# A threshold mask moved from a Pool compare to an Activation Sign and a Relu, with w_out split on Activation and Pool, and the first tiles and loads reordered

## The chip, the cores and the metric

One core of a Trainium2 chip. The metric is the device time in microseconds (us). TensorE is called PE here, VectorE DVE, ScalarE ACT, GpSimd Pool, and SP is the engine that only starts transfers.

## The reference, cut to what matters

Three layers follow each other: attention in which each row keeps its 32 largest scores, a dense layer pair with a parametric Relu, and a layer of eight experts of which each token takes two.

```
scores = scale * np.matmul(q, k.transpose(0, 1, 3, 2))          # (2, 8, 576, 576)
kth = np.partition(scores, -32, axis=-1)[..., -32:-31]
scores = np.where(scores >= kth, scores, -1e9)
attn = exp(scores - max); attn /= attn.sum(-1) + 1e-9
x = (attn @ v), heads beside each other                         # (1152, 512)
h = x @ w_in                                                    # w_in (512, 2048)
g = np.maximum(h, 0.0) + alpha * np.minimum(h, 0.0)
x = g @ w_out                                                   # w_out (2048, 512)
logits = x @ w_gate; noise_scale = log1p(exp(x @ w_noise))      # 8 experts
out = for each token: its two best experts, weight * (relu(x @ w1[e]) @ w2[e])
```

All is float32.

## The kernel before

**Stages.** The 1152 tokens are nine blocks of 128. In the first stage (to about 466 us) the program walks through 72 tiles: tile 8 * blk + h is head h of block blk, 128 rows by 576 scores. Behind it the routing is worked out and rows are scattered to their experts; the last stage (from about 530 us) runs the experts. The change touches the first stage only.

**One tile.** PE multiplies queries and keys into PSUM (`score_tile`, five tiles ahead of the rest), each number as a high and a low part. ACT copies the scores out (`copy_scores`). DVE works on pairs of tiles (`topk_pair`): four times MAX8 and three times MATCH_REPLACE8 for each tile, interleaved, and one small operation for the negated maxima (`neg_max`). ACT takes exp (`exp_tile`). Pool makes the mask `scores >= top[31]` (L1432) and multiplies it into the exponentials (L1434), both in `probabilities`. PE transposes the product in five pieces (`prob_transpose`, L846 and L848), ACT copies the pieces (`copy_prob_t`), and PE multiplies them with v (`prob_values`, L862). `row_sums` on DVE and `normalise` on Pool divide.

**The dense layers between.** While block blk is in attention, block blk - 1 goes through w_in (`first_layer`, at h = 1 to 4), back transposes (`h_transpose`), the parametric Relu and w_out (`second_layer`, at h = 5, 6, 7 and at h = 0 of the next block), in four chunks of 512. For each chunk ACT takes Relu of the negated and of the plain value (`relu_both`), scales the negated one by minus alpha with four operations of 128 columns (L1193), Pool adds the two (`prelu`, L1447), ACT rounds the sum to its high part (`high_g`), and Pool subtracts (`low_g`, L1452). `prelu` stands at h = 4, 5, 6, 7 of Pool's order.

**Order.** Every engine has its own order, written out by hand as a loop over h = 0 to 7 for each block; blocks 0 to 4 and 8 are written out, 5 to 7 are a loop. Semaphores are the only tie. An engine that waits holds back all that is queued behind it. The scores have eight buffers, exponentials, maxima and thresholds four.

**w_out's parts.** In block 1 DVE splits w_out into high and low, a quarter behind each of the four pairs (`split_w_out`, L389 and L391). w_in is loaded once PE has four tiles of scores, w_out once it has eight.

## Time and profile before

| | us |
|---|---|
| median of 3 runs | 786.79 (786.48 to 788.63) |
| the profiled execution | 789.1 |
| its span | 787.3 |
| mean granted PE clock | 0.952 of full speed |
| busy: PE, DVE, ACT, Pool | 688.5, 567.0, 435.2, 421.4 |

The profile is one execution. A slice of a line of tenths is 19.7 us. "Idle before" is what an engine stood still before an instruction, and behind the arrow stands what released it. The start of a tile's last transpose (L848) marks its place on PE: tile 8 at 70.18, tile 16 at 127.29, tile 24 at 178.33, tile 32 at 228.89, tile 40 at 284.00, tile 48 at 331.16, tile 56 at 378.39, tile 64 at 425.56, tile 71 at 465.66. Blocks thus take 57.1, 51.0, 50.6, 55.1, and then 47.2 us each.

### The profile page before, as it was taken

How to read it: one execution, taken by the hardware profiler on the slowest of the kernel's cores; microseconds unless marked ns; L12 is line 12 of the kernel's file. 1: busy time of each engine (PE TensorE's matmuls, PEld its weight loads, DVE VectorE, ACT ScalarE, POOL GpSimd, SP SyncE). 2: the span in 40 equal slices, each digit the busy share in tenths (PEclk: the TensorE clock that was granted, in tenths of full speed). 3: DMA queues.
4: the chain of work that ended last, by engine and by line, in shares of the span. 5: the costliest groups of instructions: out<-in, count | busy, mean ns of one | idle time of the engine just before them, and what ended most of it. 6: DMA issues, size and time to landing. Idle time of an engine off the chain costs nothing. (4 is left out here: it accounts for less than half of the span.)

```text
span 787.3 us, 13289 instructions
## 1 busy us (share of the span) xinstructions
PE 688.5 (87%) x4516; PEld 534.7 (68%) x4516; DVE 567.0 (72%) x1168; ACT 435.2 (55%) x863; POOL 421.4 (54%) x309
## 2 busy tenths in 40 slices
PE   2565788989999999999999989729999999999993
PEld 2454466667675676766667566518989999999893
DVE  5999999989897889897998904653555545555520
ACT  6643464756885758667666645722535535535511
POOL 3875788697776796978879770630202102112022
PEclk9968899999998999999999999958999999999998
DMA  7595001403402504040160205355267376375322
GB/s 230 211 363 226 15 14 55 148 14 120 129 26 65 165 15 149 14 161 13 60 234 13 95 17 198 135 205 183 69 212 219 115 226 193 121 246 161 121 34 33
DMA packets 36718, 98.87 MB, mean 126 GB/s; under 512 B 10480, under 2 KB 11504, under 8 KB 35184
## 3 DMA queue, kind: packets, MB, share of 16 engines
q1 hardware_dynamic: 32288, 88.31, 32.2%
q0 software_dynamic: 4384, 9.98, 5.7%
q8 instruction: 25, 0.41, 0.2%
q14 instruction: 21, 0.17, 0.1%
HBM read 80.15 MB, written 37.34 MB: 149 GB/s over the span
## 5 line engine op out<-in xcount | busy, mean ns | idle before, releaser
L1432 POOL TENSOR_SCALAR scores<-scores,top 128x576 f32<-128x576 f32 x72 | 129.0, 1792 | 78.1 <-issue 31.9
L1530 POOL DMA_INDIRECT out_dram<-ye,xe x24 | 42.8, 1783 | 216.8 <-ACT ye L1354 211.9
L364 DVE MAX8 top<-rest 128x8 f32<-128x576 f32 x216 | 151.9, 742 | 0.0
L884 PE MATMUL bank<-w_in_sb,x_t 128*128 128x512 f32 x272 | 125.9, 606 | 0.3
L1434 POOL TENSOR_TENSOR expo<-scores,expo 128x576 f32<-128x576 f32 x72 | 107.7, 1496 | 6.0
L370 DVE MATCH_REPLACE8 rest<-top,rest 128x576 f32<-128x576 f32 x144 | 105.4, 737 | 0.0
L912 PE MATMUL bank<-w_out_high,g_parts 128*128 128x512 f32 x288 | 99.3, 406 | 1.2 <-DVE g_parts L566 0.8
L1058 PE MATMUL bank<-w_hi,he_t 128*128 128x512 f32 x256 | 91.9, 400 | 0.0
L573 DVE TENSOR_TENSOR w_lo<-raw,w_hi 128x1024 fp32r<-128x1024 f32 x64 | 77.9, 1225 | 19.5 <-ACT w_hi L1301 18.6
L884 PEld LDWEIGHTS bank<-w_in_sb,x_t 128*128 128x128 f32 x272 | 50.3, 195 | 52.0 <-issue 51.1
L846 PE MATMUL bank<-ident,expo 128*128 128x128 f32 x288 | 49.9, 299 | 36.8 <-POOL expo L1434 30.6
L862 PEld LDWEIGHTS bank<-v,prob_t 128*64 128x64 f32 (+1 forms) x1440 | 56.3, 142 | 37.8 <-issue 25.2
L364 DVE MAX8 top<-scores 128x8 f32<-128x576 f32 x72 | 50.9, 748 | 31.8 <-POOL expo L1434 18.6
L1131 ACT COPY prob_t<-bank 128x512 f32<-128x512 f32 x72 | 42.4, 589 | 56.4 <-PE bank L848 56.3
L862 PE MATMUL bank<-v,prob_t 128*64 128x65 f32 (+1 forms) x1440 | 71.7, 238 | 1.5 <-ACT prob_t L1132 1.4
L809 PE MATMUL ps_scores<-k_parts,q_high 128*128 128x288 f32 x160 | 57.4, 372 | 17.2 <-DVE q_low L441 6.3
L1044 PE MATMUL ps_scores<-xe_t,w_hi 128*128 128x320 f32 x320 | 71.4, 310 | 0.0
L1301 ACT CAST w_hi<-raw 128x1024 fp32r<-128x1024 f32 x64 | 66.3, 1045 | 0.2
L846 PEld LDWEIGHTS bank<-ident,expo 128*128 128x128 f32 x288 | 33.3, 150 | 46.7 <-POOL expo L1434 25.3
L912 PEld LDWEIGHTS bank<-w_out_high,g_parts 128*128 128x128 f32 x288 | 55.5, 193 | 13.8 <-POOL g_parts L1452 1.8
L625 DVE SCALAR_TENSOR_TENSOR he_t<-ps_scores,he_t 128x64 fp32r<-128x64 f32 x80 | 22.2, 320 | 52.8 <-ACT he_t L1347 52.8
L1347 ACT ACTIVATE he_t<-ps_scores 128x320 fp32r<-128x320 f32 x40 | 17.5, 439 | 76.2 <-PE ps_scores L1044 76.2
(178 smaller groups left out, 1505.9 us busy)
## 6 DMA issues: line engine op xcount, KB each, us to landing
raw<-w_dram SPq DMA_DIRECT2D x64, 512.0 KB, 9.5
x_sorted_dram<-x_sorted_dram SPq DMA_DIRECT2D x7, 2570.0 KB, 10.8
q_raw<-q_rows_dram SPq DMA_DIRECT2D x18, 256.0 KB, 2.6
xe<-x_sorted_dram SPq DMA_DIRECT2D x8, 514.0 KB, 4.3
w_in_sb<-w_in_dram SPq DMA_DIRECT2D x4, 1024.0 KB, 8.3
w_out_raw<-w_out_dram SPq DMA_DIRECT2D x4, 1024.0 KB, 8.6
out_dram<-x_now SPq DMA_DIRECT2D x1, 3584.0 KB, 30.1
x_sorted_dram<-x_now SPq DMA_DIRECT2D x1, 2570.0 KB, 20.5
```

Of the source, the lines that this page charges most:

```text
L364: nc.vector.max(dst, src).then_inc(chain if r < ROUNDS - 1 else dve_top, 1)
L370: nc.vector.match_replace(rest[:, k, :], top[:, (n + k) % 4, 8 * r:8 * r + 8], src, LOWEST).then_inc(chain, 1)
L573: nc.vector.tensor_tensor(w_lo[par][:, at], raw[par][:, at], w_hi[par][:, at].bitcast(F32), ALU.subtract).then_inc(dve_wl, 1)
L846: pe.transpose(ps_pt[:, kt * P:(kt + 1) * P], expo[:, h % 4, kt * P:(kt + 1) * P], ident[:, :])
L862: mm = pe.matmul(ps_o[lo:hi, c:c + VCOLS], prob_t[0:n, h % 2, kt * P + lo:kt * P + hi], v[0:n, head, kt, :], start=(kt == 0), stop=(kt == ...
L884: mm = pe.matmul(dst, x_t[:, k, :], w_in_sb[:, k, c * 512:(c + 1) * 512], start=(k == 0), stop=(k == MK - 1))
L912: mm = pe.matmul(ps_y[:, :], g_parts[:, c % 2, a, k * P:(k + 1) * P], w[:, at], start=(c == 0 and k == 0 and a == 0 and w is w_out_high), ...
L1044: mm = pe.matmul(h_bank[m % 3][:, 0:GROUP], w[:, k, at], xe_t[:, a, k, :], start=(k == 0 and a == 0 and w is w1_hi), stop=(k == MK - 1 and ...
L1058: mm = pe.matmul(y_bank[t][:, :], he_t[:, m, at:at + P], w[:, m, :], start=(m == 0 and a == 0 and w is w2_hi), stop=(m == EK - 1 and a == 1))
L1301: nc.scalar.copy(w_hi[par][:, at], raw[par][:, at]).then_inc(act_wh, 1)
L1432: nc.gpsimd.tensor_scalar(mask, mask, top[:, n % 4, TOPK - 1:TOPK], None, ALU.is_ge).then_inc(pool_mask, 1)
L1434: nc.gpsimd.tensor_tensor(expo[:, n % 4, :], mask, expo[:, n % 4, :], ALU.mult).then_inc(pool_prob, 1)
```

## The change

- **Mask.** Pool works out, once for each pair of tiles, minus the next number below the 32nd largest score (`thresholds`: two small tensor_scalar and two small tensor_tensor, three waits between them). ACT writes Sign(score - that number) over the scores (`sign_tile`), for tiles h + 1 and h + 2 at odd h, right behind `copy_prob_t`. Pool keeps one multiplication for a tile; the product is negative where the mask is out. `copy_prob_t` uses Relu in place of Copy, so these become 0.
- **exp.** ACT issues exponentials in pairs at even h, for tiles h + 2 and h + 3.
- **Parametric Relu.** The four scalings by minus alpha move from ACT to Pool, ahead of the addition in `prelu`.
- **w_out.** The high parts are ACT casts at tiles 2 to 9, the low parts Pool subtractions at tiles 5 to 12, in eighths. DVE has none.
- **DVE.** `neg_max` and the row sums' addition become tensor_tensor with a constant operand. A pair starts with its first tile's scores, and waits no longer for Pool's product, but for ACT's exp and for the thresholds of the pair two before it.
- **Start.** Queries are loaded first and cast on DVE; ACT's order in the first tiles changes, and the first exponentials come earlier.
- **Loads.** w_out is loaded at once behind v, w_in when PE has eight tiles of scores, and alpha, gates and noise behind w_in.

```
-                wait(dve, pool_prob, tile - 2)
+                dve.wait_ge(act_scores, tile + 1)
+                wait(dve, act_exp, tile - 2)
+                wait(dve, pool_thr, pairs - 1)
...
-                        nc.vector.tensor_scalar(neg_max[:, m:m + 2], top[:, m:m + 2, 0], -1.0, None,
-                                                ALU.mult).then_inc(dve_negmax, 1)
+                        nc.vector.tensor_tensor(neg_max[:, m:m + 2], zeros[:, :], top[:, m:m + 2, 0],
+                                                ALU.subtract).then_inc(dve_negmax, 1)
...
-                    if split:
-                        split_w_out(pair)
...
+            def high_w_out(c):
+                act.wait_ge(w_out_in[c // 2], 16)
+                at = slice(c * 2 * MODEL, (c + 1) * 2 * MODEL)
+                nc.scalar.copy(w_out_high[:, at], w_out_raw[:, at]).then_inc(act_w_high, 1)
+
+            def sign_tile(tile, n, pairs):
+                act.wait_ge(pool_thr, pairs)
+                act.wait_ge(act_exp, tile + 1)
+                nc.scalar.activation(scores[:, n % SBUFS, :], scores[:, n % SBUFS, :], ACT.Sign,
+                                     bias=neg_below[:, n % 4:n % 4 + 1]).then_inc(act_sign, 1)
...
-                for k in range(4):
-                    ins = nc.scalar.activation(neg[:, c % 2, k, :], neg[:, c % 2, k, :], ACT.Copy,
-                                               scale=neg_alpha[:, 4 * c + k:4 * c + k + 1])
-                ins.then_inc(act_scaled, 1)
...
+                    if h % 2 and not (last and h + 2 >= HEADS):
+                        sign_tile(tile + 1, h + 1, PAIRS * blk + (h + 1) // 2 + 1)
+                        sign_tile(tile + 2, h + 2, PAIRS * blk + (h + 1) // 2 + 1)
...
+            def thresholds(n, pairs):
+
+                pool.wait_ge(dve_top, 2 * pairs)
+                plain(pool)
+                m = n % 4
+                thr = top[:, m:m + 2, TOPK - 1]
+                nc.gpsimd.tensor_scalar(step_up[:, :], thr, NEXT, 0.0, ALU.mult, ALU.max).then_inc(pool_step, 1)
+                nc.gpsimd.tensor_scalar(step_down[:, :], thr, -NEXT, TINY, ALU.mult, ALU.max).then_inc(pool_step, 1)
+                pool.wait_ge(pool_step, 3 * pairs - 1)
+                nc.gpsimd.tensor_tensor(step_up[:, :], step_up[:, :], step_down[:, :], ALU.add).then_inc(pool_step, 1)
+                pool.wait_ge(pool_step, 3 * pairs)
+                wait(pool, act_sign, 2 * pairs - 4)
+                nc.gpsimd.tensor_tensor(neg_below[:, m:m + 2], step_up[:, :], thr, ALU.subtract).then_inc(pool_thr, 1)
+                pool.wait_ge(pool_thr, pairs)
...
-                mask = scores[:, n % SBUFS, :]
-                nc.gpsimd.tensor_scalar(mask, mask, top[:, n % 4, TOPK - 1:TOPK], None, ALU.is_ge).then_inc(pool_mask, 1)
-                pool.wait_ge(pool_mask, tile + 1)
-                nc.gpsimd.tensor_tensor(expo[:, n % 4, :], mask, expo[:, n % 4, :], ALU.mult).then_inc(pool_prob, 1)
+                pool.wait_ge(act_sign, tile + 1)
+                nc.gpsimd.tensor_tensor(expo[:, n % 4, :], scores[:, n % SBUFS, :], expo[:, n % 4, :],
+                                        ALU.mult).then_inc(pool_prob, 1)
...
-                pool.wait_ge(act_scaled, 4 * j + c + 1)
+                pool.wait_ge(act_relu, 4 * j + c + 1)
+                plain(pool)
+                for k in range(4):
+                    ins = nc.gpsimd.tensor_scalar(neg[:, c % 2, k, :], neg[:, c % 2, k, :],
+                                                  neg_alpha[:, 4 * c + k:4 * c + k + 1], None, ALU.mult)
+                ins.then_inc(pool_scaled, 1)
+                pool.wait_ge(pool_scaled, 4 * j + c + 1)
                 nc.gpsimd.tensor_tensor(pos[:, c % 2], pos[:, c % 2], neg[:, c % 2], ALU.add).then_inc(pool_g, 1)
...
+                    if isinstance(blk, int) and HEADS * blk + h in W_LOW_AT:
+                        low_w_out(W_LOW_AT[HEADS * blk + h])
+                    if h % 2 and not (last and h == HEADS - 1):
+                        thresholds(h + 1, PAIRS * blk + (h + 1) // 2 + 1)
```

DVE between two pairs of block 1, before. `top` holds the largest scores of a row, `rest` the scores with those struck out.

```order
L364 MAX top<-rest 128x8 [waits chain] x2
L389 CAST w_out_high<-w_out_raw 128x2048 [waits w_out_in]
L391 TENSOR_TENSOR w_out_low<-w_out_raw,w_out_high 128x2048 [waits dve_w_high]
L364 MAX top<-scores 128x8 [waits pool_prob,act_scores]
L364 MAX top<-scores 128x8
L370 MATCH_REPLACE rest<-top,scores 128x576 [waits chain] x2
L374 TENSOR_SCALAR neg_max<-top 128x2
```

And the same place after:

```order
L378 MAX top<-rest 128x8 [waits chain] x2
L378 MAX top<-scores 128x8 [waits pool_thr,act_scores,act_exp]
L378 MAX top<-scores 128x8 [waits act_scores]
L384 MATCH_REPLACE rest<-top,scores 128x576 [waits chain] x2
L388 TENSOR_TENSOR neg_max<-zeros,top 128x2
```

The split is gone, and the pair waits for `pool_thr` and `act_exp` in place of `pool_prob`.

Pool at h = 5 and the start of h = 6 of block 1, before; the same order stands in every later block. `expo` are the exponentials, `pos` and `neg` the two halves of the parametric Relu, `g_parts` its high and low part.

```order
L1432 TENSOR_SCALAR scores<-scores,top 128x576 [waits dve_top,act_exp]
L1434 TENSOR_TENSOR expo<-scores,expo 128x576 [waits pool_mask]
L1452 TENSOR_TENSOR g_parts<-pos,g_parts 128x512 [waits act_g_high]
L1447 TENSOR_TENSOR pos<-pos,neg 128x512 [waits act_scaled]
L1432 TENSOR_SCALAR scores<-scores,top 128x576 [waits dve_top,act_exp]
```

And after:

```order
L1469 TENSOR_TENSOR expo<-scores,expo 128x576 [waits act_sign]
L1500 TENSOR_TENSOR g_parts<-pos,g_parts 128x512 [waits act_g_high]
L1491 TENSOR_SCALAR neg<-neg,neg_alpha 128x128 [waits act_relu]
L1491 TENSOR_SCALAR neg<-neg,neg_alpha 128x128 x3
L1495 TENSOR_TENSOR pos<-pos,neg 128x512 [waits pool_scaled]
L1443 TENSOR_SCALAR step_up<-top 128x2 [waits dve_top]
L1444 TENSOR_SCALAR step_down<-top 128x2
L1446 TENSOR_TENSOR step_up<-step_up,step_down 128x2 [waits pool_step]
L1449 TENSOR_TENSOR neg_below<-step_up,top 128x2 [waits act_sign,pool_step]
L1469 TENSOR_TENSOR expo<-scores,expo 128x576 [waits act_sign,pool_thr]
```

One large operation has gone, and four scalings and four threshold operations have come; the next multiplication waits for `act_sign`.

ACT at h = 5 of a block in the loop, before (`h_sb` and `prob_t` are copies out of PSUM):

```order
L1156 COPY h_sb<-bank 128x512 [waits pe_ht1,pe_first]
L1131 COPY prob_t<-bank 128x512 [waits pe_pv,pe_pt]
L1132 COPY prob_t<-bank 64x128
L1200 CAST g_parts<-pos 128x512 [waits pe_second,pool_g]
```

And after:

```order
L1180 COPY h_sb<-bank 128x512 [waits pe_ht1,pe_first]
L1154 ACTIVATE prob_t<-bank 128x512 [waits pe_pv,pe_pt]
L1155 ACTIVATE prob_t<-bank 64x128
L1135 ACTIVATE scores<-scores,neg_below 128x576 [waits act_exp,pool_thr] x2
L1217 CAST g_parts<-pos 128x512 [waits pe_second,pool_g]
```

Two Signs, which wait for the thresholds, stand between the copies and the cast that Pool's `low_g` waits for.

## Rows read from the trace of the kernel before

**Rows 1.** The page, busy tenths of PE and its granted clock in 40 slices:
```profile
PE   2565788989999999999999989729999999999993
...
PEclk9968899999998999999999999958999999999998
```

**Rows 2.** Stretches between last transposes: length, PE, PEld, DVE, ACT, POOL busy, clock, DMA:
```profile
70.18:99.80 29.62, 24.40 (x154) 15.50 (x153) 29.55 (x52) 14.84 (x34) 19.41 (x11) 0.84 0.04 14
99.80:127.29 27.49, 23.23 (x170) 17.25 (x168) 27.38 (x50) 16.00 (x36) 24.41 (x17) 0.94 0.03 11
...
331.16:354.16 23.00, 22.92 (x166) 15.00 (x165) 22.81 (x48) 15.09 (x35) 17.97 (x14) 1.00 0.38 138
354.16:378.39 24.23, 23.05 (x182) 17.25 (x181) 20.02 (x42) 16.85 (x39) 20.76 (x16) 1.00 0.03 11
```

**Rows 3.** Timeline of DVE, block 1: start, us, operation, idle before:
```profile
53.92 1.42 DVE L364 MAX8 top<-scores 128x8 f32<-128x576 f32 x2
...
64.15 1.47 DVE L389 CAST w_out_high<-w_out_raw 128x2048 fp32r<-128x2048 f32 x1
65.65 2.29 DVE L391 TENSOR_TENSOR w_out_low<-w_out_raw,w_out_high 128x2048 fp32r<-128x2048 f32 x1
...
112.94 1.42 DVE L364 MAX8 top<-scores 128x8 f32<-128x576 f32 x2
```

**Rows 4.** Timeline of DVE, the pairs of the first block that waited:
```profile
11.44 1.42 DVE L364 MAX8 top<-scores 128x8 f32<-128x576 f32 x2 [2.85 <-ACT scores L1095]
...
32.80 1.42 DVE L364 MAX8 top<-scores 128x8 f32<-128x576 f32 x2 [1.84 <-ACT scores L1095]
```

**Rows 5.** Groups of Pool from 331.16 to 378.39: busy us, mean ns, idle before:
```profile
L1432 POOL TENSOR_SCALAR scores<-scores,top 128x576 f32<-128x576 f32 x8 | 13.8, 1726 | 7.0 <-issue 4.2 <-ACT expo L1125 2.9
L1434 POOL TENSOR_TENSOR expo<-scores,expo 128x576 f32<-128x576 f32 x8 | 11.3, 1417 | 0.7
L1452 POOL TENSOR_TENSOR g_parts<-pos,g_parts 128x512 fp32r<-128x512 f32 x5 | 6.4, 1281 | 0.5 <-ACT g_parts L1200 0.5
L1447 POOL TENSOR_TENSOR pos<-pos,neg 128x512 f32<-128x512 f32 x4 | 5.2, 1289 | 0.0
```

**Rows 6.** Small Pool operations of the whole span, and ACT's exp, same columns:
```profile
L1387 POOL TENSOR_SCALAR_AFFINE_SELECT ident<-ident 128x128 f32<-128x128 f32 x1 | 0.3, 284 | 0.2 <-POOL ident L1385 0.2
L1475 POOL TENSOR_TENSOR neg_alpha<-below,alpha_sb 128x16 f32<-128x16 f32 x1 | 0.2, 210 | 0.0
...
L1125 ACT ACTIVATE expo<-scores,neg_max 128x576 f32<-128x576 f32 x72 | 55.5, 772 | 0.0
```

**Rows 7.** Timelines of Pool and DVE where small operations of one met the other:
```profile
86.05 1.72 POOL L1432 TENSOR_SCALAR scores<-scores,top 128x576 f32<-128x576 f32 x1
86.27 0.54 DVE L374 TENSOR_SCALAR neg_max<-top 128x2 f32<-128x2 f32 x1
...
338.09 1.41 POOL L1434 TENSOR_TENSOR expo<-scores,expo 128x576 f32<-128x576 f32 x1
338.55 0.97 DVE L374 TENSOR_SCALAR neg_max<-top 128x2 f32<-128x2 f32 x1
...
504.00 0.61 POOL L1511 COPY x<-weight 128x7 f32<-128x7 f32 x1 [2.82 <-DMA x_sorted_dram<-x,slot_i]
503.33 2.36 DVE L573 TENSOR_TENSOR w_lo<-raw,w_hi 128x1024 fp32r<-128x1024 f32 x2
```

**Rows 8.** Timeline of PE and ACT at tile 55 (h = 7):
```profile
371.90 0.66 PE L846 MATMUL bank<-ident,expo 128*128 128x128 f32 x4 [0.89 <-POOL expo L1434]
372.39 0.27 PE L848 MATMUL bank<-ident,expo 128*64 128x128 f32 x1
372.70 0.59 ACT L1131 COPY prob_t<-bank 128x512 f32<-128x512 f32 x1 [1.07 <-PE bank L848]
373.19 0.26 ACT L1132 COPY prob_t<-bank 64x128 f32<-64x128 f32 x1
```

**Rows 9.** Timeline of SP, the issue of w_out's four pieces:
```profile
38.46 2.52 SPq L704 DMA_DIRECT2D w_out_raw<-w_out_dram  x4
```

More of the change, by code:

```diff
@@ L86 @@
 K_LOW_AFTER = {12: (0, 1), 15: (2, 3), 16: (4, 5), 17: (6, 7)}
+W_HIGH_AT = {2 + c: c for c in range(8)}
+W_LOW_AT = {5 + c: c for c in range(8)}
 OTHER_AT = {MIXED * HEADS - AHEAD + i: i for i in range(HEADS)}
@@ L208, in moe_program @@
         dve_k_high = sem("dve_k_high")
-        act_q = [sem(f"act_q{i}") for i in range(2)]
+        q_high_ready = [sem(f"q_high_ready{i}") for i in range(2)]
         q_ready = [sem(f"q_ready{i}") for i in range(2)]
@@ L216, in moe_program @@
         w_in_in = sem("w_in_in")
-        w_out_in = sem("w_out_in")
+        w_out_in = [sem(f"w_out_in{i}") for i in range(4)]
         small_in = sem("small_in")
@@ L346, in _, with topk_pair @@
         def _(dve):
-            def topk_pair(tile, n, mixed=False):
+            def topk_pair(tile, n, pairs, mixed=False):
                 pair = n // 2
-                for k in range(2):
-                    dve.wait_ge(act_scores, tile + k + 1)
-                    if mixed:
-                        dve.wait_ge(act_other, n + k + 1)
-                wait(dve, pool_prob, tile - 2)
+                dve.wait_ge(act_scores, tile + 1)
+                wait(dve, act_exp, tile - 2)
+                wait(dve, pool_thr, pairs - 1)
                 plain(dve)
@@ L361, in topk_pair @@
                             dve.wait_ge(chain, LINKS * pair + 4 * r - 1 + k)
+                        elif k:
+                            dve.wait_ge(act_scores, tile + 2)
+                        if r == 0 and mixed:
+                            dve.wait_ge(act_other, n + k + 1)
+                        if r == 0 and k:
+                            plain(dve)
                         src = rest[:, k, :] if r else scores[:, n + k, :]
@@ L414, in one_block @@
                         row_sums(blk - 1, 0)
-                    if split:
-                        split_w_out(pair)
-                    if pair == (0 if split else 1) and not first:
+                    if pair == (0 if second else 1) and not first:
                         row_sums(blk - 1, 1)
@@ L443, in _ @@
             first_low_keys(1)
+            dve.wait_ge(small_const, 2)
             one_block(0, True)
-            one_block(1, split=True)
+            one_block(1, second=True)
             one_block(2)
@@ L1130, in copy_prob_t @@
                 wait(act, pe_pv, tile - 1)
-                nc.scalar.copy(prob_t[:, n % 2, 0:(KT - 1) * P], ps_pt[:, :])
-                nc.scalar.copy(prob_t[0:LASTK, n % 2, (KT - 1) * P:], ps_pt4[0:LASTK, 0:P]).then_inc(act_pt, 1)
+                nc.scalar.activation(prob_t[:, n % 2, 0:(KT - 1) * P], ps_pt[:, :], ACT.Relu)
+                nc.scalar.activation(prob_t[0:LASTK, n % 2, (KT - 1) * P:], ps_pt4[0:LASTK, 0:P],
+                                     ACT.Relu).then_inc(act_pt, 1)
             def copy_o(blk, n):
@@ L1243, in one_block @@
                         relu_both(blk - 1, TURN_AT[h])
-                    if not (last and h + 2 >= HEADS):
+                    if h % 2 == 0 and not (last and h + 2 >= HEADS):
                         exp_tile(tile + 2, h + 2, PAIRS * blk + (h + 2) // 2 + 1)
+                        exp_tile(tile + 3, h + 3, PAIRS * blk + (h + 2) // 2 + 1)
+                    if isinstance(tile, int) and tile in W_HIGH_AT:
+                        high_w_out(W_HIGH_AT[tile])
                     if isinstance(tile, int) and tile in OTHER_AT:
@@ L1259, in _ @@
             high_keys(0)
-            high_queries(0, 0)
             high_keys(1)
@@ L1273, in _ @@
             high_keys(7)
-            for tile in range(2):
-                exp_tile(tile, tile, 1)
+            sign_tile(0, 0, 1)
+            sign_tile(1, 1, 1)
             one_block(0, mlp=False, gate=False)
@@ L1419, in _ @@
                     pool.wait_ge(q_ready[1], 1)
+                if h == 5:
+                    thresholds(0, 1)
             pool.wait_ge(v_in_first, 32)
```

86 lines of the change are left out of this document (48 added, 38 removed).

## The prediction

> **What bounds the kernel now.** I read the page's tenths first: PE fills all slices but a dip near 500 us from the fifth or sixth on, and the early ones are thin [rows 1]. So the question is which engine holds PE up in which stretch, and the stretches between transposes answer it [rows 2]. In block 1 (70.18 to 127.29, 57.1 us) DVE is busy 29.55 of 29.62 and 27.38 of 27.49 us, while PE does its work at a granted clock of 0.84 and 0.94: DVE bounds. In a block of the loop (331.16 to 378.39, 47.2 us) PE is busy 22.92 of 23.00 and 23.05 of 24.23: PE bounds, and all that a better order can give back is 1.3 us a block. 0.89 of it is one wait, at h = 7, for Pool's product [rows 8]. The second half of that block, h = 4 to 7, is also Pool's fullest: 20.76 of 24.23 us against 17.97 of 23.00 in the first [rows 2]. The change eases DVE and loads just this half.
>
> **The start: -2 us.** The first pair now begins with one tile's scores. Its wait of 2.85 us was for two [rows 4]; the second tile still comes when it came, so one MAX8 of 0.7 us is gained. Pair 2 waited 1.84 us for scores [rows 4], which hung on the first products. Those no longer need the 1.73 us compare, and the exponentials are there earlier. I take all of it: the fifth pair starts at 53.92 [rows 3] less 1.95, 52.0. Bounds are 0 and -2.5.
>
> **Block 1 on DVE.** The four splits cost 1.47 + 2.29 each [rows 3], 15.0 us together, all on the bound, and they go. From 53.92 to 112.94 DVE then needs 59.0 - 15.0 = 44.0 us, 10.6 to 11 a pair: pairs end at 62.7, 73.6, 84.4 and 95.8. If DVE alone counted, tile 16 would be 17 us early.
>
> **neg_max: nothing.** It took 0.97 us when it met Pool's multiply, and ended with it; beside the compare it took 0.54 and ended 0.76 us after the compare began [rows 7]. One could hope that tensor_tensor is free of that. But a Pool copy of 7 elements took 0.61 us while a DVE tensor_tensor ran [rows 7], so I leave the waits in. The Trainium skill says the same of such operations (SBUF: State Buffer, section Who interferes with whom): one with two SBUF inputs contends with a GpSimd instruction that reads SBUF. By that rule the new form waits as the old one did. Were it free, block 1's DVE would end about 1.5 us earlier, and Pool (below) would hide it.
>
> **What Pool gets.** These prices decide.
> - Compare out: 1.73 us a tile, 13.8 us a block [rows 5].
> - Scaling in: 16 tensor_scalar of 128 columns a block. The trace has none. By columns from the compare (1.73 for 576, taken as 0.1 fixed and 2.8 ns a column) one is 0.46 us. Bounds: 0.28, what a one-input 128x128 took [rows 6]; and 1.13, if what the compare did after it let DVE through at 0.76 us (0.97 us more [rows 5, 7]) is a fixed tail: 0.97 + 128/576 of 0.76. I take 0.46, since a tail that long beside 0.28 is odd. One `prelu` goes from 1.29 [rows 5] to 3.13 us.
> - Thresholds in: four operations of two columns, as 0.21 for 16 columns [rows 6], 0.85 us a pair. Bounds 0.4 and, with the fixed tail, 2.4.
> - w_out's low parts in: 1024 columns, twice the 1.28 of 512 [rows 5], 2.55 us, eight times, tiles 5 to 12. The high parts go to ACT, which is busy 14.84 of 29.62 us there [rows 2]: nothing.
>
> **A new wait.** Pool's multiply for an even tile needs ACT's Sign (0.77 as exp [rows 6]), and that needs Pool's thresholds, queued behind `prelu`. With hand-overs, Pool stands still about 0.95 us, before the multiplies of h = 6 and of the next h = 0. On ACT, copy_scores, Relu and the cast for `low_g` are queued behind the waiting Sign; DVE has its scores five tiles ahead, so it does not feel this.
>
> **Block 1 on Pool.** Pair 6 (tile 12) is done at 84.4, thresholds 85.2, Sign 86.2, multiply 87.6. Then Pool has, until tile 16's multiply is done: four `prelu` 12.5, four multiplies 5.7 [rows 5], three `low_g` 3.8, one query part 1.3, the last w_out part 2.55, two thresholds 1.7, two gaps 1.9. Sum 29.5: 117.1. The transposes (0.49 to the start of the last [rows 8]) put tile 16's mark at 117.6 instead of 127.29: **-9.7**. PE's own need from tile 12 on is 23 us [rows 2], so Pool bounds, not DVE.
>
> **Each later block.** PE from tile 3's mark to the next block's tile 0 (h = 4 to 7 and one more step) takes 30.2 us today. After: ACT begins its copies 0.31 behind the mark and needs 0.8 for them [rows 8], then signs tile 4, so Pool's multiply starts 2.0 us behind the mark. From its start to the end of the next tile 0's multiply there are five multiplies 7.1, four `prelu` 12.5, three `low_g` 3.8, query part 1.3, thresholds 1.7, and idle 0.3 + 0.95 + 0.95: 28.6. With the transposes, 31.1, and the block takes 47.2 + 0.9 = 48.1. PE's wait of 0.89 at h = 7 goes to h = 0 and is about twice as long. So:
> - block 2 (tile 16 to 24): 51.0 to 48.1, **-2.9**;
> - blocks 3 and 4 (105.7 us with scores of the second batch, which stretch PE's steps and hide Pool): DVE was late there; **-2**, between -5 and +2;
> - four blocks of 47.2, with the last one shorter: 3.3 x 0.9, **+3**.
>
> **The rest.** w_in is now issued when w_out was, at 38.46 [rows 9]; it is wanted at tile 8, past 62, and w_out's early issue is 30 us ahead of use: nothing, unless a load takes over 20 us. Table and copies with Relu in place of Copy: nothing. The routing and the experts move with tile 71: 0. At the end one `prelu` more of 1.8 us meets a multiply that is 1.1 earlier: 0 to +1.
>
> **Sum.** -9.7 - 2.9 - 2 + 3 = -11.6. Against the profiled execution's 789.1 that is 777.5; against the median of 786.79, which is 0.3% below it, **775.2**.
>
> **Rivals.**
> - *Scaling is costly on Pool* (slower). The price of one 128-column tensor_scalar decides: each 0.1 us more is 1.6 us in the chain of a block, for eight blocks 13 us. From 0.55 us on nothing is gained, and at 0.75 the time is 775 + 38 = 813; with the fixed tail of 1.13 Pool would be busy far beyond 47 us a block, and the time past 860. For it: the compare released DVE at 0.76 and still ran to 1.73 [rows 7]. Against: 0.28 for a one-input 128x128 [rows 6].
> - *Scaling is cheap on Pool* (faster). The compare may be slow as a comparison; a multiplication would then be near 0.28. `prelu` is 2.4 us, a block 46.9, tile 16 comes at 115, limited by PE. -12 - 4 - 3 - 1 = -20: 767. The Trainium skill points here (GPSIMD Engine Reference, section 4.1): one-input operations are roughly line-rate, two-input ones about half as fast. The trace disagrees for the compare, 1.73 against 1.42 of the two-input multiply [rows 5]. Taken fully, it would be this rival's lower end, 762.
> - *The early gain is lost on the way*: tile 16 only 4 us earlier, as ACT's waiting Sign holds up copies or PE's clock stays at 0.84 [rows 2]. 775.2 + 5.7 = 781.
> - That the change does not do what it says is excluded for the splits: their rows are gone from DVE's order.
>
> **Chances.** Forecast (scaling at 0.38 to 0.54) 0.42; cheap 0.18; early gain lost 0.06; costly 0.34. About 0.3% is what a measurement here can tell from no change; of the forecast 0.04 lies within that, and of each of the last two 0.02. Of the lost gain another 0.02 ends slower. So faster 0.38 + 0.18 + 0.02 = 0.58, within 0.08, slower 0.32 + 0.02 = 0.34. The range leaves out some 5% below and 15% above, where the scaling costs over 0.69 us: 763 to 805.
>
> **What would show it.** Right: tile 16's mark at 117 to 118, L1491 at 0.46 us, Pool 24 to 25 us busy in h = 4 to 7, PE's wait at h = 0 on Pool's product, blocks of the loop near 48.1, DVE's neg_max as long as before, the span of the experts unchanged. Wrong: L1491 above 0.55 (the block passes 50) or near 0.3 (PE busy without a gap), or neg_max at 0.15 throughout, or a Sign that waits on DVE.

## The result, and the profile after

The changed kernel takes 830.06 us (median of 4 runs, 826.67 to 830.31) against 787.29 us of the kernel before in the same session: a ratio of 1.0531, 95% interval 1.0500 to 1.0563. It is slower by 5.3%, where 775.2 us and "faster" had been forecast. The profiled execution took 826.67 us, its span is 824.9 us against 787.3.

The page of the changed kernel, the same two lines as in [rows 1], and the shares of its chain that ended last:

```profile
PE   2455987989879989889899898945999999999994
...
PEclk9965899989989999999999999975999999999998
...
PE 48%; POOL 25%; issue 10%; DVE 7%; ACT 6%; DMA 2%; POOLq 0%; SPq 0%; ACTq 0%; DVEq 0%
```

Pool now stands in a quarter of the chain, though it is busy for only 414.0 of 824.9 us. The starts of the last transposes tell where the 37.6 us between the two spans arose. The forecast's steps stand beside them (us, change against the kernel before):

| stage | before | after | forecast | measured |
|---|---|---|---|---|
| to tile 8 | 70.18 | 67.26 | -2 | -2.9 |
| block 1 (tile 8 to 16) | 57.1 | 64.0 | -7.7 | +6.9 |
| block 2 | 51.0 | 54.6 | -2.9 | +3.6 |
| blocks 3 and 4 | 105.7 | 114.9 | -2 | +9.2 |
| blocks 5 to 8, to tile 71 | 181.7 | 199.0 | +3 | +17.3 |
| behind tile 71 | 321.6 | 325.1 | 0 | +3.5 |
| sum | | | -11.6 | +37.6 |

Every stage behind the start came out worse. Stretches between last transposes of the changed kernel, with the columns of [rows 2]: block 1 in two halves, then one block of the loop (51.7, 53.4 and 51.8 us instead of 47.2):

```profile
67.26:101.63 34.37, 24.86 (x153) 15.72 (x152) 33.22 (x65) 16.90 (x32) 20.49 (x23) 0.76 0.11 41
101.63:131.25 29.62, 23.15 (x170) 17.09 (x169) 22.23 (x45) 16.57 (x33) 26.97 (x34) 0.94 0.03 10
...
352.52:378.64 26.12, 24.72 (x166) 16.20 (x165) 20.62 (x44) 15.44 (x32) 12.94 (x21) 0.93 0.33 121
378.64:405.91 27.27, 24.64 (x182) 18.52 (x181) 21.03 (x45) 17.05 (x35) 24.59 (x33) 0.94 0.03 10
```

Pool is busy 24.59 of 27.27 us in the second half, as forecast (24 to 25), but only 12.94 of 26.12 in the first, where PE, at a lower granted clock, is busy 24.72. That looks like a chain that goes from engine to engine, not like one full engine. The groups of Pool and DVE (busy, mean ns, idle before), answering to [rows 5 to 7]:

```profile
L1469 POOL TENSOR_TENSOR expo<-scores,expo 128x576 f32<-128x576 f32 x72 | 101.9, 1416 | 103.6 <-ACT scores L1135 103.5
L1491 POOL TENSOR_SCALAR neg<-neg,neg_alpha 128x128 f32<-128x128 f32 x128 | 78.9, 637 | 0.0
...
L388 DVE TENSOR_TENSOR neg_max<-zeros,top 128x2 f32<-128x2 f32 x36 | 12.8, 355 | 0.0
L394 DVE TENSOR_TENSOR den<-o_sb,least 128x4 f32<-128x4 f32 x18 | 13.6, 758 | 39.0 <-ACT o_sb L1169 37.6 <-ACT o_sb L1165 1.2
```

Two things show: one scaling takes 0.637 us and not 0.46, and Pool waits 103.5 us in all for ACT's Signs. (That sum alone is no measure of the loss: it is 109.7 us in the 773 us kernel further down.) Pool's timeline in the loop (start, us, operation, idle before) shows the long form of that wait, at tile 52 (h = 4), and the short one at tile 56 (h = 0):

```profile
365.92 0.20 POOL L1449 TENSOR_TENSOR neg_below<-step_up,top 128x2 f32<-128x2 f32 x1 [0.16 <-POOL step_up L1446]
374.46 1.42 POOL L1469 TENSOR_TENSOR expo<-scores,expo 128x576 f32<-128x576 f32 x1 [8.35 <-ACT scores L1135]
375.86 2.38 POOL L1491 TENSOR_SCALAR neg<-neg,neg_alpha 128x128 f32<-128x128 f32 x4
378.32 1.29 POOL L1495 TENSOR_TENSOR pos<-pos,neg 128x512 f32<-128x512 f32 x1
379.57 1.42 POOL L1469 TENSOR_TENSOR expo<-scores,expo 128x576 f32<-128x576 f32 x1
...
401.89 0.24 POOL L1443 TENSOR_SCALAR step_up<-top 128x2 f32<-128x2 f32 x1
402.87 0.20 POOL L1449 TENSOR_TENSOR neg_below<-step_up,top 128x2 f32<-128x2 f32 x1 [0.16 <-POOL step_up L1446]
403.96 1.41 POOL L1469 TENSOR_TENSOR expo<-scores,expo 128x576 f32<-128x576 f32 x1 [0.89 <-ACT scores L1135]
```

The thresholds of tile 52 are there at 366.1, but its Sign stands behind tile 51's `copy_prob_t` in ACT's order, so Pool idles 8.35 us and starts its whole chain only then. That start was foreseen: 1.8 us behind tile 51's mark at 372.66, forecast 2.0. From the product of tile 52 to the end of that of tile 56 it takes 405.37 - 374.46 = 30.9 us; the forecast had put 28.6 there. PE's waits in the same block:

```profile
352.03 0.66 PE L855 MATMUL bank<-ident,expo 128*128 128x128 f32 x4 [2.15 <-POOL expo L1469]
...
362.71 1.55 PE L893 MATMUL bank<-w_in_sb,x_t 128*128 128x512 f32 x3 [1.40 <-ACT x_t L1175]
...
397.02 0.66 PE L855 MATMUL bank<-ident,expo 128*128 128x128 f32 x4 [1.81 <-POOL expo L1469]
405.42 0.66 PE L855 MATMUL bank<-ident,expo 128*128 128x128 f32 x4 [0.82 <-POOL expo L1469]
```

The wait of 1.40 us for `x_t` is new and was in no step of the forecast. ACT's timeline says whose it is: two Signs stand ahead of the copies.

```profile
360.14 1.43 ACT L1135 ACTIVATE scores<-scores,neg_below 128x576 f32<-128x576 f32 x2
361.47 0.63 ACT L1104 ACTIVATE scores<-ps_scores 128x576 f32<-128x576 f32 x1
362.00 0.57 ACT L1175 COPY x_t<-bank 128x512 f32<-128x512 f32 x1
```

And a wait can cost more than its length. Behind the wait of 2.15 us, PE's granted clock fell to its lower level, 1.2 GHz, for a few us (windows, columns as above):

```profile
354.00:356.60 2.60, 2.60 (x8) 1.99 (x7) 2.14 (x6) 2.05 (x4) 2.35 (x5) 0.50 0.01 3
357.00:359.18 2.18, 2.18 (x29) 1.62 (x27) 2.18 (x8) 0.59 (x1) 0.00 (x0) 1.00 0.00 0
...
352.52:359.18 6.66, 6.66 (x44) 5.13 (x42) 5.97 (x15) 3.76 (x8) 4.03 (x8) 0.74 0.01 2
405.91:410.99 5.08, 5.08 (x44) 3.98 (x43) 4.38 (x10) 3.75 (x8) 4.05 (x8) 1.00 0.00 0
```

The step of h = 0 took 6.66 us there, without a gap, and 5.08 one block later, after a wait of only 0.82 us. So the fall behind the wait of 2.15 us cost another 1.6: this block takes 20.14 us to tile 3's mark, the blocks before and behind it 18.55. The length of a wait does not decide by itself: behind the 1.81 us at 397.02 the clock was 0.50 from 398 to 401, but behind another wait of 1.81 us, at 343.73, it stayed at 1.00, as it did behind the 1.40 us at 362.71.

In block 1 two chains stand out. The first one, at the start of the block (Pool, ACT, DVE):

```profile
60.58 2.37 POOL L1475 TENSOR_TENSOR w_out_low<-w_out_raw,w_out_high 128x1024 fp32r<-128x1024 f32 x1
64.03 1.44 ACT L1135 ACTIVATE scores<-scores,neg_below 128x576 f32<-128x576 f32 x2 [1.24 <-POOL neg_below L1449]
66.84 0.37 ACT L1169 COPY o_sb<-bank 128x260 f32<-128x260 f32 x1
67.25 1.94 DVE L394 TENSOR_TENSOR den<-o_sb,least 128x4 f32<-128x4 f32 x1 [4.66 <-ACT o_sb L1169]
69.45 1.42 DVE L378 MAX8 top<-scores 128x8 f32<-128x576 f32 x2
```

The thresholds stand behind a subtraction for w_out on Pool, the Signs wait for the thresholds, the copy of tile 7's output is queued behind the Signs and a w_out cast of ACT, and DVE's row sum waits 4.66 us for it. Pair 5 starts at 69.45, as before (69.48): the start's gain and the first split that went from DVE are both lost to this wait. The second one comes at tile 10:

```profile
81.61 1.44 ACT L1135 ACTIVATE scores<-scores,neg_below 128x576 f32<-128x576 f32 x2 [5.12 <-POOL neg_below L1449]
84.12 5.28 PE L893 MATMUL bank<-w_in_sb,x_t 128*128 128x512 f32 x8 [6.02 <-ACT x_t L1175]
```

Here a Sign waits for thresholds that wait for DVE's pair (7.09 us on Pool), and PE waits 6.02 us for a copy that stands behind it.

### The profile page after: what moved, and what is told of

It is laid out like the page before. It is cut to its first block, busy times and chain, and to the rows that moved or that the text cites. A ratio compares the mean times of both kernels' runs of the same rounds, so it can differ in the third digit from the quotient of the medians.

```text
span 824.9 us, 13626 instructions
## 1 busy us (share of the span) xinstructions
PE 701.7 (85%) x4516; PEld 545.4 (66%) x4516; DVE 551.2 (67%) x1163; ACT 452.5 (55%) x814; POOL 414.0 (50%) x517
## 4 chain that ended last, share of the span: by engine, by line
PE 48%; POOL 25%; issue 10%; DVE 7%; ACT 6%; DMA 2%; POOLq 0%; SPq 0%; ACTq 0%; DVEq 0%
PE bank L1067 11%; POOL neg L1491 9%; PE ps_scores L1053 9%; PE bank L893 6%; POOL expo L1469 6%; PE bank L1053 5%; PE bank L921 5%; POOL pos L1495 4%; PE bank L1072 4%; POOL g_parts L1500 3%; DVE top L378 3%; DVE rest L384 3%; ACT scores L1135 3%; PE bank L855 2%; PE bank L871 2%
## 5 line engine op out<-in xcount | busy, mean ns | idle before, releaser
L1469 POOL TENSOR_TENSOR expo<-scores,expo 128x576 f32<-128x576 f32 x72 | 101.9, 1416 | 103.6 <-ACT scores L1135 103.5
L1582 POOL DMA_INDIRECT out_dram<-ye,xe x24 | 42.8, 1783 | 217.3 <-ACT ye L1378 212.5
L893 PE MATMUL bank<-w_in_sb,x_t 128*128 128x512 f32 x272 | 124.7, 602 | 15.6 <-ACT x_t L1175 15.6
L921 PE MATMUL bank<-w_out_high,g_parts 128*128 128x512 f32 x288 | 106.5, 433 | 1.7 <-POOL g_parts L1500 0.8
L384 DVE MATCH_REPLACE8 rest<-top,rest 128x576 f32<-128x576 f32 x144 | 105.7, 740 | 0.0
L378 DVE MAX8 top<-scores 128x8 f32<-128x576 f32 x72 | 53.5, 754 | 61.9 <-ACT scores L1104 49.0
L1135 ACT ACTIVATE scores<-scores,neg_below 128x576 f32<-128x576 f32 x72 | 51.8, 767 | 50.0 <-POOL neg_below L1449 50.0
L1491 POOL TENSOR_SCALAR neg<-neg,neg_alpha 128x128 f32<-128x128 f32 x128 | 78.9, 637 | 0.0
L921 PEld LDWEIGHTS bank<-w_out_high,g_parts 128*128 128x128 f32 x288 | 60.1, 209 | 17.3 <-POOL g_parts L1500 3.2
L921 PE MATMUL bank<-w_out_low,g_parts 128*128 128x512 f32 x144 | 60.7, 422 | 0.0
```

The source lines that it names most:

```text
L378: nc.vector.max(dst, src).then_inc(chain if r < ROUNDS - 1 else dve_top, 1)
L384: nc.vector.match_replace(rest[:, k, :], top[:, (n + k) % 4, 8 * r:8 * r + 8], src, LOWEST).then_inc(chain, 1)
L893: mm = pe.matmul(dst, x_t[:, k, :], w_in_sb[:, k, c * 512:(c + 1) * 512], start=(k == 0), stop=(k == MK - 1))
L921: mm = pe.matmul(ps_y[:, :], g_parts[:, c % 2, a, k * P:(k + 1) * P], w[:, at], start=(c == 0 and k == 0 and a == 0 and w is w_out_high), ...
L1135: nc.scalar.activation(scores[:, n % SBUFS, :], scores[:, n % SBUFS, :], ACT.Sign, bias=neg_below[:, n % 4:n % 4 + 1]).then_inc(act_sign, 1)
L1469: nc.gpsimd.tensor_tensor(expo[:, n % 4, :], scores[:, n % SBUFS, :], expo[:, n % 4, :], ALU.mult).then_inc(pool_prob, 1)
```

## Experiments

Two theories were tested first. **P**: Pool's price, 0.637 instead of 0.46 us for each of 128 scalings. **A**: ACT's order, in which a Sign that waits for thresholds holds up `copy_scores`, `copy_x_t` and `copy_o`. The first four kernels ran beside the kernel before at 786.70 us, the next four at 786.13, the last four at 786.84.

**The scalings back on ACT**, the rest of the change kept.

```
-                    ins = nc.gpsimd.tensor_scalar(neg[:, c % 2, k, :], neg[:, c % 2, k, :],
-                                                  neg_alpha[...], None, ALU.mult)
+                    ins = nc.scalar.activation(neg[:, c % 2, k, :], neg[:, c % 2, k, :], ACT.Copy,
+                                               scale=neg_alpha[...])
```

> The changed kernel with one part undone: the four scalings by minus alpha stand on ACT again, as before; Sign, thresholds and all else stay. Theory P (Pool's price): the loss is the scaling on Pool, 16 x 0.637 us a block in the half block in which Pool is fullest; without it Pool has 14.4 us there instead of 24.6 and the blocks of the loop fall from 53 us to PE's own 46 to 47.5; time 775 to 788. Theory A (ACT's order): the loss is the Sign that waits for the thresholds and holds up copy_x_t, copy_scores and copy_o; it stays and ACT gets 5 us a block more; time 810 to 830.

Measured 786.94 us, ratio 0.9992 (0.9980 to 1.0004): 43.1 us less than the whole change. That is P's range, though the loop's blocks take 47.9 to 48.1 us where P had said 46 to 47.5. But 787 is no gain on the kernel before, so what the change had to gain is still being eaten by something else.

**The scaling as one instruction.** Four `tensor_scalar` of 128 columns become one `tensor_tensor` of 512 with minus alpha broadcast.

```
-                for k in range(4):
-                    ins = nc.gpsimd.tensor_scalar(...)
+                nc.gpsimd.tensor_tensor(neg[:, c % 2], neg[:, c % 2],
+                                        neg_alpha[:, 4 * c:4 * c + 4].unsqueeze(2).to_broadcast([P, 4, P]),
+                                        ALU.mult).then_inc(pool_scaled, 1)
```

> The changed kernel with the four tensor_scalar of 128 columns of a chunk replaced by one tensor_tensor of 512 columns on Pool, minus alpha broadcast; by the two-input rows 1.28 us in place of 2.38, so Pool's chain of h = 4 to 7 is 4.4 us shorter. Theory P: 4 us a block over eight blocks, as far as PE lets it, time 797 to 805. Theory A: little of it is on the path, 820 to 828.

Measured 793.71 us, ratio 1.0081 (1.0058 to 1.0103). Its group of Pool:

```profile
L1490 POOL TENSOR_TENSOR neg<-neg,neg_alpha 128x512 f32<-128x512 f32 x32 | 34.1, 1066 | 0.0
```

One takes 1.07 us for four of 2.37 together, 1.3 us less in each of 32 places or 42 us of Pool's time, and the kernel gained 36.3. By the instruction of the old form that is 0.33 us less for 36.3 us, 11 us for each 0.1 us, close to the forecast's 13. The time is 3 us below P's range. It also says how much the price can explain: four scalings now cost what 0.27 us for each would, less than the 0.46 of the forecast, and the kernel is still 18.5 us above the forecast's 775.2.

**The Signs behind the copies.** They move behind `copy_scores` and `copy_x_t` in ACT's order.

```
                     copy_prob_t(tile, h)
-                    if h % 2 ...: sign_tile(tile + 1, ...); sign_tile(tile + 2, ...)
...
                     if mlp and h == 1:
                         copy_x_t(blk - 1)
+                    if h % 2 ...: sign_tile(tile + 1, ...); sign_tile(tile + 2, ...)
```

> The changed kernel with the two Signs of odd h moved in ACT's order, from right behind copy_prob_t to behind the cast for low_g, copy_scores and copy_x_t. Theory A: PE's waits of 1.4 us a block for copy_x_t and DVE's 49 us of waits for scores go, time 805 to 818. Theory P: Pool's products come 0.6 to 1.3 us later twice a block, and the chain with the scaling bounds as before; 828 to 840.

Measured 808.93 us, ratio 1.0272 (1.0252 to 1.0293): 21.1 us less, A's range. The waits (total, times, longest) of the changed kernel, then of this one:

```profile
ACT scores L1135 <- POOL neg_below L1449: 50.0, 19, 5.1
DVE top L378 <- ACT scores L1104: 49.0, 24, 5.2
PE bank L855 <- POOL expo L1469: 33.4, 17, 7.5
PE bank L893 <- ACT x_t L1175: 15.6, 8, 6.0
```

```profile
POOL expo L1469 <- ACT scores L1135: 97.6, 35, 6.9
DVE top L378 <- ACT scores L1104: 56.3, 25, 7.1
PE bank L855 <- POOL expo L1469: 35.4, 18, 7.5
```

PE's wait for `x_t` has gone from the list, ACT's own wait for thresholds has fallen from 50.0 to 3.3 us, and PE's wait for Pool's product has stayed. DVE's waits for scores, which A had expected to go, grew from 49.0 to 56.3 us while the kernel became 21.1 us faster: they were not what it lost time by. So both theories hold, each for its part, and A's part is above all the copy that PE waits for.

**The mask back on Pool**, with the scalings still there. Thresholds and Signs go, Pool compares again.

```
-                pool.wait_ge(act_sign, tile + 1)
-                nc.gpsimd.tensor_tensor(expo[...], scores[...], expo[...], ALU.mult).then_inc(pool_prob, 1)
+                nc.gpsimd.tensor_scalar(mask, mask, top[:, n % 4, TOPK - 1:TOPK], None, ALU.is_ge).then_inc(pool_mask, 1)
+                pool.wait_ge(pool_mask, tile + 1)
+                nc.gpsimd.tensor_tensor(expo[...], mask, expo[...], ALU.mult).then_inc(pool_prob, 1)
```

> The changed kernel with the mask undone: Pool compares again, there are no thresholds and no Sign; the scaling stays on Pool, and the w_out split, loads, pairs of exponentials and DVE's tensor_tensor stay. Theory P: Pool in h = 4 to 7 goes from 24.6 us busy plus its gaps of 2 us to 24.6 - 1.9 + 4 x 1.73 = 29.6 us, so a block takes 55 to 57 us and the time is 845 to 870. Theory A: with the Signs gone ACT never waits for Pool's thresholds; 795 to 815.

Measured 816.30 us, ratio 1.0363 (1.0333 to 1.0393). That is far below P's range and 1 us above A's. P had said that taking the compare off Pool was worth 15 us and more; in truth it made the kernel 14 us slower, although Pool was rid of 1.73 us a tile. So P alone does not explain the change; A does so here, since the mask from ACT brings its order along.

**Neither scaling nor mask**: the two edits above undone together. What remains is w_out's split on ACT and Pool, the start, the loads, the paired exponentials and DVE's two small `tensor_tensor`.

> The change without its two large parts: the mask is Pool's compare again and the scalings are ACT's again; the split of w_out on ACT and Pool, the order of the first tiles and loads, the paired exponentials and DVE's two tensor_tensor stay. Theory one (what DVE gives up in block 1 is real, and was eaten by the two large parts): tile 16's mark comes 4 to 10 us before the 127.3 of the kernel before, the loop's blocks are 47.2 again: 777 to 783. Theory two (block 1 has a second bound just behind DVE: the queries of block 2 land late and Pool now carries eight casts of 2.4 us): tile 16 at 125 to 128, 785 to 789.

Measured 773.50 us, ratio 0.9829 (0.9798 to 0.9860), faster than either theory had said. Tile 16's mark is at 121.50, the loop's blocks take 46.5 us.

**Queries ahead of the blank rows**, in the whole change.

```
+            next_queries(2, [0])
             sp.dma_start(out[:, :]..., x2_now...).then_inc(out_blank, 16)
-            next_queries(2)
+            next_queries(2, [1])
```

> The whole change, with one edit: SyncE issues block 2's queries ahead of the blank rows of the output instead of behind them, the first half ahead, the second behind. In block 1 of the changed kernel ACT waits 3.9 us for these queries at 72.4, as the last to come. Theory one (the reordered loads cost block 1 this wait): tile 16's mark 3 to 5 us earlier, 825 to 827. Theory two (the wait stands in the shadow of Pool and of the Sign behind it): tile 16 within 1 us of 131.3, 829 to 831.

Measured 829.98 us, ratio 1.0553 (1.0523 to 1.0583), tile 16 at 131.46: nothing, as theory two said. That the wait lies in the shadow of the next Sign fits (PE's wait for `x_t` is 6.0 us at the longest, as before), but is not shown by itself.

**Scalings on ACT and Signs late**: the first and third edits together.

> The scalings on ACT (as in the first run) and the Signs behind the copies in ACT's order (as in the third). If both causes are the ones, and independent, the 43 us and the 21 us they gave alone meet the floor that PE sets: loop blocks of 46.5 to 47.9, no wait of PE for copy_x_t, 776 to 784. If the late Sign costs as much as it gives once Pool has room (PE then waits for Pool's product), 785 to 790, and the wait for copy_x_t is gone while the one for the product has grown.

Measured 773.01 us, ratio 0.9816 (0.9783 to 0.9849). That is 3 us below the range for two independent causes. The loop's blocks take 46.6 to 46.8 us, and PE is busy 45.60 of 46.62 us: with both causes removed PE bounds the loop again. Its timeline of a whole block of the loop has one wait, not for Pool:

```profile
348.50 0.66 PE L906 MATMUL bank<-ident,h_sb 128*128 128x128 f32 x4 [0.94 <-ACT h_sb L1181]
```

And Pool waits for ACT's Signs as long as ever, where it costs nothing:

```profile
POOL expo L1477 <- ACT scores L1136: 109.7, 35, 6.1
```

**The same with the queries ahead.**

> As the run before in this call, with block 2's first queries issued ahead of the blank rows. If the queries are a bound of block 1 once Pool is relieved: tile 16's mark 3 to 5 us earlier than there, and the time 3 to 5 us shorter. If Pool's casts of w_out bound block 1 instead, less than 1 us.

Measured 770.51 us, ratio 0.9790 (0.9750 to 0.9829), the fastest kernel of this study. Its interval overlaps that of the run before, so the 2.5 us alone would prove nothing; but tile 16's mark moved from 119.94 to 117.60, less than the 3 to 5 us expected, and ACT's wait of 6.21 us for the queries is gone.

**A list of prices on Pool.** In the whole change, only the first of a block's four groups keeps its scalings. The others do this:

```
+                if c == 3:
+                    ins = nc.gpsimd.tensor_scalar(neg[:, c % 2], neg[:, c % 2], -0.25, None, ALU.mult)
...
+                    elif c == 1:
+                        ins = nc.gpsimd.tensor_scalar(neg[:, c % 2, k, :], neg[:, c % 2, k, :], -0.25, None, ALU.mult)
+                    else:
+                        ins = nc.gpsimd.tensor_copy(neg[:, c % 2, k, :], neg[:, c % 2, k, :])
```

> A list of prices on Pool. The whole change, but of a block's four groups of scalings only the first is left as it is (four tensor_scalar of 128 columns, factor from a column of SBUF); the second multiplies by the constant -0.25 in four instructions, the third copies the four 128-column pieces onto themselves, the fourth multiplies all 512 columns by -0.25 in one instruction. So minus alpha is applied in the first group alone. Theory one (a fixed part of each instruction and a price by the column: a line through 0.637 us for 128 and the compare's 1.74 for 576 has 0.32 + 2.46 ns a column): the constant 128-column form 0.60 to 0.65 us, the 512-column one 1.5 to 1.65, the time 818 to 826 against 830. Theory two (the factor read from SBUF is what costs): the constant form 0.25 to 0.45, the 512-column one 0.6 to 1.2, the time 790 to 812. The copy: 0.28 as for a one-input operation of the kernel before, or as the constant form.

Measured 811.66 us, ratio 1.0319 (1.0291 to 1.0347). Groups of Pool, in this order: factor from SBUF, constant, constant with 512 columns, copy.

```profile
L1494 POOL TENSOR_SCALAR neg<-neg,neg_alpha 128x128 f32<-128x128 f32 x32 | 18.9, 607 | 0.0
L1497 POOL TENSOR_SCALAR neg<-neg 128x128 f32<-128x128 f32 x32 | 17.1, 559 | 0.7
L1491 POOL TENSOR_SCALAR neg<-neg 128x512 f32<-128x512 f32 x8 | 12.4, 1551 | 0.7
...
L1500 POOL COPY neg<-neg 128x128 f32<-128x128 f32 x32 | 8.2, 298 | 0.0
```

The constant form fits a fixed part and a price by the column: (1551 - 559) / 384 = 2.58 ns a column and 0.23 us fixed. Reading the factor from SBUF adds 0.05. So theory one holds for the price, though 0.559 lies a little below the 0.60 it had named. The compare is not slow as a comparison: 0.23 + 0.05 + 576 columns at 2.58 ns make 1.77 us, and it took 1.73. Only the copy is cheap, 0.298, and so was the one-input operation that had bounded the forecast's price from below [rows 6]. The time, 811.66, is below theory one's 818 to 826 and inside theory two's 790 to 812; it is the prices that decide against theory two. Why the time came out lower was not looked into.

**w_out's splits back on DVE**, in the kernel of only the rest (`split_w_out(pair)` again in block 1, `high_w_out` and `low_w_out` gone).

> The kernel of only_rest, with w_out's four splits back on DVE in block 1 and nothing of w_out on ACT and Pool. The difference from only_rest is what the moved splits are worth, the difference from the kernel before is what the start, the loads, the paired exponentials and DVE's small tensor_tensor are worth. If the moved splits make block 1's gain: tile 16's mark at 125 to 127, loop blocks as in only_rest (46.5), 777 to 781. If the order makes it: tile 16 at 121 to 123 and 773 to 775.

Measured 781.10 us, ratio 0.9929 (0.9912 to 0.9947), tile 16 at 126.62, loop blocks 46.5. That is the case in which the splits make block 1's gain. So the moved splits are worth 7.6 us, and the rest of the reordering 5.7 us, of which 0.7 us in each block of the loop.

**Queries ahead, in the kernel of only the rest.**

> The kernel of only_rest, with block 2's first queries issued ahead of the blank rows of the output. With the mask on ACT the same edit moved tile 16's mark by 2.0 us net of the start and the time by 2.5. Here ACT waits 3.4 us for these queries in block 1. If the queries hold the scores that DVE wants next, 2 to 3 us: 770 to 772. If Pool (compare, product and casts of w_out) bounds block 1 here, less than 1 us: 773 to 774.

Measured 774.28 us, ratio 0.9831 (0.9814 to 0.9847): nothing gained against 773.50, as was expected if Pool bounds block 1 there. Between the marks Pool is busy 49.12 of 52.10 us in the kernel without this edit:

```profile
69.40:121.50 52.10, 45.72 (x321) 32.24 (x320) 45.07 (x98) 32.33 (x71) 49.12 (x32) 0.88 0.05 19
```

**DVE's two small operations as tensor_tensor**, alone in the kernel before.

```
-                        nc.vector.tensor_scalar(neg_max[...], top[...], -1.0, None, ALU.mult)
+                        nc.vector.tensor_tensor(neg_max[...], zeros[:, :], top[...], ALU.subtract)
```

> The kernel before, with DVE's two small tensor_scalar operations (minus the row's maximum, the row sum plus 1e-9) as tensor_tensor, and nothing else. If tensor_tensor waits for Pool's compare and product as the old form did, as I forecast: mean near 0.58 us, longest near 1.2, 785 to 788, loop blocks 47.2. If it is free of Pool: mean 0.15, tile 16's mark 1 to 2 us earlier, 783 to 786, and loop blocks nearer 46.5.

Measured 787.56 us, ratio 1.0000 (0.9988 to 1.0012). The group, against x36 | 20.8, 578 for the old form in the kernel before:

```profile
L377 DVE TENSOR_TENSOR neg_max<-zeros,top 128x2 f32<-128x2 f32 x36 | 20.8, 578 | 0.0
```

The same mean to the nanosecond. The 355 ns in the changed kernel is not the new form's doing: the same form takes 664 ns with compare and scalings both moved back (only the rest), 398 with the compare on Pool and the scalings there too, and 207 with Signs late and scalings on ACT. It goes with what Pool runs beside it.

The times of the two big edits, with all else of the change in place (us):

| scalings | mask on Pool | Sign ahead of the copies | Sign behind the copies |
|---|---|---|---|
| on ACT | 773.50 | 786.94 | 773.01 |
| on Pool | 816.30 | 830.06 | 808.93 |

Down each column the scalings on Pool cost 42.8, 43.1 and 35.9 us. Along each row, early Signs cost 13.4 and 13.8 us against the mask on Pool. Late Signs gain 0.5 and 7.4: nothing where PE bounds already, something where Pool does. Scalings and early Signs add up against the mask on Pool. Not quite so for moving the Signs: it gives 21.1 us with the scalings on Pool and 13.9 with them on ACT, so some 7 us are common to both causes. The columns differ in Pool's compare as well as in ACT's order, so only the last two compare the order alone.

## Why the prediction was wrong, point by point

**What bounds: right.** DVE bound block 1 and PE the loop. Without scalings and early Signs the loop's blocks fall from 47.2 to 46.5 us, about half of the 1.3 us that I had called the most an order can give back.

**The start, -2: right in size, lost on the way.** Tile 8's mark came 2.9 us earlier, pair 4 on DVE 1.5 (52.38), but pair 5 not at all. The step took DVE's time as the only thing between the pairs and forgot the row sum in between, which needs tile 7's output. Before, the first split of w_out stood ahead of it and hid that wait; with the splits back on DVE, in the kernel of only the rest, it is gone again. The wait is 4.66 us here, 4.10 in the fastest kernel, whose late Signs still stand ahead of that copy, and 2.89 without any Sign. Even in the fastest kernel pair 4 to pair 5 takes 65.83 - 51.10 = 14.7 us, where I had 10.7.

**Block 1, -9.7 at tile 16's mark: the steps were right in another kernel.** I had put the mark at 117.6. The fastest kernel, with scalings on ACT and Signs late, has it at 117.60, the one of only the rest at 121.50. The agreement is partly luck, since the first has no scalings on Pool and the forecast had. In the changed kernel the mark is at 131.25. That Pool and not DVE would bound fits (26.97 busy of 29.62 us in the second half, DVE 22.23). The splits cost 15.0 us on the bound, and moving them was worth 7.6.

**Pool's price for a scaling: the first step that failed.** I took 0.46 us by a line through the compare with 0.1 us fixed. The fixed part is 0.23, and the factor's read comes on top: 0.637 on average. From one scaling's start to the end of its `prelu` it is 3.71 us (375.86 to 379.57), not 3.13, 0.58 more in each of four a block. These 2.3 us are all that Pool's chain was longer than forecast (30.9 against 28.6). By the rule of 13 us for 0.1 us, the 0.18 us are 23 us; by the 0.58, 0.58 x 4 x 8 = 19 us. So the rival with the costly scaling had the direction right, but not the size: at 0.637 its rule gives 798, 32 us below the 830. Nor was 0.55 the point from which nothing is gained: at the equivalent of 0.27, in one instruction, the kernel with early Signs took 793.7 us, still no gain. The rule of one-input work at roughly line-rate (the Trainium skill, GPSIMD Engine Reference, section 4.1) can hold here for the copy at most, of which one size was run: a multiplication by a constant, also of one input, took 0.559 us for the same 128 columns and 1.551 for 512, more than a two-input `tensor_tensor` of that size (1.29 in [rows 5]).

**"DVE has its scores five tiles ahead, so it does not feel this": the second step that failed.** The text had named part of what is queued behind the waiting Sign, and then counted it at nothing. As said, it is wrong: DVE's waits for scores came to 49.0 us in 24 places, before to 5.8 in 2. But these waits grew when the Signs were moved and the time fell, so what the runs show as loss lies with a member of the queue that the step left out: `copy_x_t`, for which PE waited 15.6 us in 8 places, 6.02 the longest. (`copy_o`, for DVE's row sum, is another, told above.) Moving the Signs behind the copies took PE's waits for `x_t` away and gave 21.1 us here, of which these waits can be 15.6, and 13.9 with the scalings on ACT. The waiting Sign was priced for h = 6 and 0 only, from Pool's side; the block's first half, which had been taken as unchanged, got 1.5 us longer, and 3.1 where the clock fell too. A block of the loop in its two halves (us between marks) sets the two steps apart:

| kernel | tile 0 to 3 | tile 3 to next tile 0 |
|---|---|---|
| before | 17.0 | 30.2 |
| forecast | 17.0 | 31.1 |
| the change | 18.6 (20.1 once) | 33.2 |
| scaling as one instruction | 18.6 | 29.2 |
| scalings on ACT | 18.3 | 29.6 |
| the same, Signs late, queries ahead | 17.0 | 29.6 |

The price acts in the second half alone, and early Signs lengthen the first half whatever the scalings cost.

**PE's clock after a wait: not in the sum.** I had asked what a wait costs PE in time. In the loop a wait of 2.15 us was followed by a step of 6.66 instead of 5.08 us. In the second half, where Pool's chain bounds, a fall of the clock cost next to nothing: 33.17 us in the block without one, 33.25 in the two with one.

**Sum.** 775.2, with 19 to 23 for the price and 14 to 21 for the order of ACT, comes to 808 to 819; the other 11 to 22 us are not shown. In blocks 5 to 8 the account closes, as an estimate: the forecast's 3, 2.1 x 3.3 = 6.9 for the price, 5.6 for four waits for `x_t` and 1.6 for the clock are 17.1 of the 17.3 us measured. In blocks 1 to 4 it does not. They came 32.3 us above the forecast, of which price and `x_t` make some 9 and 10; the other 13, with the clock and tile 8's hand-over among them, stay open, and so does the tail (+3.5, where the kernels with scalings on ACT have 321 to 322 us behind tile 71 and those with four scalings on Pool 323 to 325).

**neg_max, nothing: right**, and so was the rule beside it, that an operation with two SBUF inputs contends with a GpSimd instruction that reads SBUF (the Trainium skill, SBUF — State Buffer, section Who interferes with whom). The trace agrees with it: 0.578 us on average in both forms, where the shortest `tensor_tensor` took 0.145 us and the longest 1.40.

**The loads, nothing: half right.** The term looked at w_in and w_out and left the queries out. The reordering made ACT wait 3.9 to 6.2 us for block 2's queries in block 1. It costs nothing where an early Sign waits anyway or Pool is full, and some 2.5 us, at the edge of what the runs can tell, where neither is so. Before, ACT waited 1.7 us for them.

**The signs named ahead.** L1491 above 0.55 and a Sign that waits on DVE both came, and the text had called either one proof that it was wrong. Pool's busy time in h = 4 to 7 fitted and told nothing.

## What to carry to other kernels

A wait that is put into an engine's queue can cost what everything behind it costs. Go through each instruction queued behind it, up to the next one that the waited-for event does not concern, and look up who waits for each of these. Then ask whether the one that waits is the bound: here DVE's waits were the longer ones, and PE's cost the time. Work that can wait belongs behind the copies that others need.

A short instruction's price on a new engine is bounded by its fixed part, so two sizes of the same operation are wanted before many short ones are moved there: here 128 instructions with a price 0.18 us off cost some 20 us. If one instruction can take their place, it should: that alone gave 36 us.

A change of five parts should be tried by its parts. This one held 1.7% of gain (773.5 us; 2.1% with Signs late, scalings on ACT and one load moved, 770.5), hidden behind two parts that cost 7% together (830.06 against 773.50).

## What the runs showed of the hardware

- On Pool, `tensor_scalar` with a constant took 0.23 us and 2.58 ns a column of 128 partitions in f32, with a factor from SBUF 0.05 us more. A copy of 128 columns took 0.298 us. A `tensor_tensor` of 512 columns took 1.29 us with two full inputs, and only 1.07 with the second one broadcast from four columns.
- A wait of PE of 2.15 us in the middle of steady work was followed by about 3 us at a granted clock of 0.50, its lower level of 1.2 GHz. Of two waits of 1.81 us one was followed by such a stretch and one was not; after waits of 1.40 and 0.82 us the clock was 1.00.
- DVE's `neg_max` on 128x2 took 578 ns on average both as `tensor_scalar` and as `tensor_tensor`, from 0.15 to 1.40 us each. Over the kernels of this study the mean of the `tensor_tensor` went from 207 to 664 ns with what Pool ran beside it.
